# The low part of the second half of an expert's relu values made in two operations, each with a count of its own

## The reference

```python
def _moe2_ref(x, modality_id, w_gate, modality_bias, w1, w2):
    ...
    e_idx = np.argmax(logits, axis=1)
    ...
    for e in range(E):
        mask = e_idx == e
        ...
        h = np.maximum(x[mask] @ w1[e], 0.0)
        out[mask] = gate_w[mask, None] * (h @ w2[e])
```

## Time and profile before

| | |
|---|---|
| median of 3 runs | 618.58 us (618.49 to 619.17) |
| the profiled execution | 619.54 us |
| its span, first to last instruction | 617.7 us |
| mean granted TensorE clock | 0.99 |
| expert stage, 415 to 617.7 us | 202.7 us |
| busy in the whole span | PE 596.2, PEld 498.0, DVE 325.4, ACT 188.1, POOL 125.1 us |
| chain that ended last, by engine | PE 86%, DVE 5%, issue 4%, ACT 2%, DMA 2% |

### The profile page before, as it was taken

How to read it: one execution, slowest core, us unless ns; L and a number is a source line. 1 busy time by engine, 2 the same in 40 slices (tenths; PEclk the granted TensorE clock), 3 DMA queues, 4 the chain that set the end, 5 groups by cost and what they waited for, 6 DMA issues and landing times.

```text
span 617.7 us, 10821 instructions
## 1 busy us (share of the span) xinstructions
PE 596.2 (97%) x3350; PEld 498.0 (81%) x3351; DVE 325.4 (53%) x814; ACT 188.1 (30%) x437; POOL 125.1 (20%) x200
## 2 busy tenths in 40 slices
PE   8999999899999999999999999999999999999996
PEld 4777777788989988899989999877777777777774
DVE  4877787687544464545644577547222228622211
ACT  4988887442010000100000220116222137521121
POOL 5444543996000000000000000010211121211120
PEclk9999999999999999999999999879999999999999
DMA  7865642463010000800010000139311117211110
GB/s 169 182 145 101 145 127 58 133 187 92 1 51 1 1 1 1 314 8 0 0 51 0 0 1 1 51 106 400 125 36 49 34 34 255 72 42 42 34 36 28
DMA packets 76588, 48.09 MB, mean 78 GB/s; under 512 B 54799, under 2 KB 62991, under 8 KB 76560
## 3 DMA queue, kind: packets, MB, share of 16 engines
q1 hardware_dynamic: 72336, 40.03, 22.4%
q0 software_dynamic: 2480, 7.34, 3.6%
q10 hardware_dynamic: 1744, 0.39, 0.3%
HBM read 41.46 MB, written 7.08 MB: 79 GB/s over the span
## 4 chain that ended last, share of the span: by engine, by line
PE 86%; DVE 5%; issue 4%; ACT 2%; DMA 2%; DVEq 1%; SPq 0%; ACTq 0%
PE wide L1160 13%; PE wide L1162 11%; PE wide L1161 11%; PE bank L1160 10%; PE bank L1162 10%; PE bank L1161 10%; PE wide L1148 9%; PE bank L1222 4%; PE wide L1202 3%; PE wide L1327 2%; PE wide L1155 1%; ACT p_sc L501 1%; DMA stage<-in_moe_w 1%; PE bank L1214 1%; DVE h_l L846 1%
## 5 line engine op out<-in xcount | busy, mean ns | idle before, releaser
L843 DVE TENSOR_SCALAR h_act<-bank,alpha_sb 128x384 f32<-128x384 f32 x62 | 38.3, 617 | 109.9 <-PE bank L1162 109.9
L1160 PE MATMUL bank<-x_hl,wts 128*128 (+1 forms) x248 | 85.3, 344 | 0.0
L1162 PE MATMUL bank<-x_hl,wts 128*128 (+1 forms) x248 | 83.5, 337 | 0.0
L1161 PE MATMUL bank<-x_hl,wts 128*128 (+1 forms) x248 | 83.3, 336 | 0.0
L1160 PE MATMUL wide<-wts,h_h 128*128 128x512 f32 x192 | 75.8, 395 | 4.1 <-DVE h_l L846 2.8
L731 POOL DMA_INDIRECT xg<-x_scratch,src_i x16 | 16.7, 1047 | 292.0 <-DVE src_i L1078 256.3
L1162 PE MATMUL wide<-wts,h_l 128*128 128x512 f32 x192 | 75.9, 395 | 0.0
L1161 PE MATMUL wide<-wts,h_h 128*128 128x512 f32 x192 | 75.7, 394 | 0.0
L1160 PE MATMUL wide<-wts,hg_h 128*128 x120 | 51.4, 428 | 5.2 <-DVE hg_l L1114 5.2
L1114 DVE TENSOR_TENSOR hg_l<-wide,hg_h 128x512 fp32r<-128x512 f32 x30 | 20.7, 690 | 64.8 <-ACT hg_h L595 48.9
L1160 PE MATMUL bank<-wts,xg_h 128*128 x120 | 48.7, 406 | 0.5 <-DVE xg_l L1102 0.5
(11 more groups left out here) (203 smaller groups left out, 1021.3 us busy)
## 6 DMA issues: line engine op xcount, KB each, us to landing
stage<-in_moe_w SPq DMA_DIRECT2D x32, 512.0 KB, 6.6
ring<-in_moe_w_in SPq DMA_DIRECT2D x16, 256.0 KB, 2.8
ring<-in_moe_w_out SPq DMA_DIRECT2D x16, 256.0 KB, 2.7
v_raw<-in_v SPq DMA_DIRECT2D x16, 192.0 KB, 2.6
x_scratch<-x2row SPq DMA_DIRECT2D x4, 768.0 KB, 3.5
k_raw<-in_k SPq DMA_DIRECT2D x14, 192.0 KB, 3.0
q_raw<-in_q SPq DMA_DIRECT2D x14, 192.0 KB, 3.3
v_win<-in_v SPq DMA_DIRECT2D x16, 120.0 KB, 2.5
```

The lines of the kernel that those rows point to most:

```text
L843: link(ts(h, acc, 0.0, alpha_sb[:, j:j + 1], ALU.min, ALU.mult))
L1160: pe.matmul(acc, lhs[0], rhs[0], start=start, stop=False)
L1161: pe.matmul(acc, lhs[0], rhs[1], start=False, stop=False)
L1162: return pe.matmul(acc, lhs[1], rhs[0], start=False, stop=stop)
```

## The change

DVE makes the low part of the second half (chunks 4 to 7) in two operations of 256 columns, and each counts `hg_low` up by one; the first half stays one operation with one count. A tile now counts three. PE waits for the first count of the second half before chunks 4 and 5, and for the second before chunks 6 and 7.

```diff
                 def hidden_low(u):
-                    part = lambda x: x[:, 4 * u:4 * u + 4].rearrange("p c t -> p (c t)")
                     dve.wait_ge(hg_high, 2 * t + 1 + u)
-                    tt(part(hg_l), wide[0][:, u * 512:(u + 1) * 512], part(hg_h).bitcast(F32), ALU.subtract
-                       ).then_inc(hg_low, 1)
+                    for c0, c1 in (((4, 6), (6, 8)) if u else ((0, 4),)):
+                        part = lambda x: x[:, c0:c1].rearrange("p c t -> p (c t)")
+                        tt(part(hg_l), wide[0][:, c0 * P:c1 * P], part(hg_h).bitcast(F32), ALU.subtract).then_inc(hg_low, 1)
...
-                pe.wait_ge(hg_low, 2 * t + 1)
+                pe.wait_ge(hg_low, 3 * t + 1)
                 down(range(2))
                 turn_h(t, 1)
                 down(range(2, 4))
-                pe.wait_ge(hg_low, 2 * t + 2)
-                down(range(4, 8))
+                pe.wait_ge(hg_low, 3 * t + 2)
+                down(range(4, 6))
+                pe.wait_ge(hg_low, 3 * t + 3)
+                down(range(6, 8))
```

## The result

| | before | changed |
|---|---|---|
| median | 618.58 us (618.37 to 619.17, 5 runs) | 615.15 us (613.60 to 616.66, 5 runs) |
| ratio | | 0.9931, 95% interval 0.9913 to 0.9948 |
| profiled execution, its span | 619.54, 617.7 us | 616.66, 614.9 us |

The change makes the kernel 3.4 us faster at the medians. Measured again, it gives 614.52 us and a ratio of 0.9924 (0.9910 to 0.9938). The forecast was 613.1 with a range of 611.6 to 616.2: the measured time lies inside it, sign and mechanism hold, and 2 us are missing.

What follows compares the result with a forecast made beforehand. PE, busy for 97% of the span, was taken as the bound, so only its waits could move the time. Gains of 3.82 at chunk 4 and 1.65 at chunk 0 make 5.5: 618.58 - 5.5 = 613.1 us, range 611.6 to 616.2.

Steps and rivals of the forecast that it cites:

- Step 1: PE's wait for chunk 4: the first count comes 0.273 earlier, 14 x 0.273 = 3.8 us gained (0 to 5.4).
- Step 2: Chunks 6 and 7 wait for a count of their own: 0.9 in hand, so no wait, 0 us.
- Step 3, chunk 0: PE's wait for chunk 0: y_copied and hg_low waited for on separate rows, 15 x 0.11 = 1.65 us gained.
- step 4: Tile of 505 to 518 us and the next: VectorE's weight splits carry the time, so the fifteenth 0.273 is lost.
- Rival B: Only the early count helps, nothing is gained at chunk 0: 614.8 us; chance 0.31.
- Step 3, PE's register work: Added register operation L1419 ahead of chunk 6 on PE: taken as 0, at most 15 x 0.11 = 1.7 us lost.
- rival C: PE's queue has no lead; three added instructions cost 0.11 each per tile, 4.95 lost, 619.7 us; chance 0.08.
- The sign that the forecast named: Mean distance of the waits for chunk 4, 13.06, falls by about 0.38 to 12.7.
- Rival D: First count seen only with the pair's end: 0.06 to 0.14 more per tile, 619.5 to 620.8 us; chance 0.03.
- Rival E: PE's loop code no longer at hand at its 14 returns: 15.0 lost, 3.8 gained, 629.8 us; chance 0.03.

Runs made afterwards that it cites:

- e1: The changed kernel, but PE waits for both counts of the second half ahead of chunk 4 and no longer ahead of chunk 6; 618.25 us.
- e3: The kernel before, with PE's wait for y_copied moved ahead of the next tile's transposes; 616.36 us, ratio 0.9955.
- e7: e6 with the wait for y_copied also moved ahead of the next tile's transposes; 610.93 us, ratio 0.9856.
- e2: The kernel before, with one added, always reached wait for hg_low ahead of chunk 6, with a register value of its own; 620.20 us, ratio 1.0016.
- e8: The kernel before, with two added, always reached waits (hg_low and e_low) ahead of chunk 6; 621.56 us.
- e0: The changed kernel run once more, no edit; 614.52 us.
- e9: e7 with the second half made in two operations, the early count on a semaphore of its own, no register instruction added; 609.69 us, ratio 0.9840.
- e6: The kernel before, with the second half's transposes behind chunk 0 instead of behind chunk 1; 612.73 us, ratio 0.9880.
- e5: The changed kernel with its early count on its own semaphore, y_copied waited for early, and operations of 128 and 384 columns; 613.20 us, ratio 0.9902.

## Why the prediction was right, and where its sizes were off

**The mechanism** held in each step that the profile could show. Step 1: the first count comes 0.27 earlier (0.420 for 256 columns where 0.417 was taken from another row of the same form); 15 distances C0 to C4 shrink by 3.99 us together, 0.266 each, against 0.273. The idle at chunk 4 is 0.34 as forecast, and e1 shows that the count alone brings it. The rule of the Trainium skill (VectorE: DVE Perf Modes, "The TRN2 errata") against small operations agrees with the trace as a price: the pair takes 0.76 instead of 0.69, and e1, where PE waits for the whole pair, pays 0.06 per tile for it. It does not decide here, because PE waits for the first part only.

**Step 2**, chunk 6 without a wait, held: no idle of the loads ahead of it.

**Step 3, chunk 0**: 0.11 per tile was taken; the 13 tiles from the second on that don't follow the tile in step 4 give 1.37 us, 0.105 each. e3 shows the cause alone: the place of the wait for `y_copied`. As built this is one instruction less behind the release. Rival B is out for the mechanism, though its 614.8 lies nearer to the medians: the time by itself could not have told it from the forecast.

**Step 3, PE's register work, is the term that was mis-sized.** I put the instruction L1419 at "0, at most 1.7 us lost", because PE issues ahead of itself and the seam's 0.14 looked like the small rest of much hidden work. It costs 0.07 per seam, 0.98 us. The seam's 0.14 was not a rest under a full cover but the sign that the cover had already run out there, since PE has stood still at chunk 4 (e7); e2 and e8 show that what is added then comes through, 0.09 for each instruction. The bound of 0.11 was right in size; to take nothing of it was the error. So rival C was partly true. Of its three instructions only this one counts: L1417 stands where PE waits, and L1413 has taken the place of another instruction and left one less behind the release.

**Step 4**: the gain at chunk 4 of the eighth tile, lost behind DVE's weight splits, is to be seen. H to C0 of the tile after it is 7.79 instead of 7.73, where all the others fell by about 0.1; from the eighth tile's C4 to this C0 it is 10.64 instead of 10.49. The rows that answer to the earlier trace rows:

```profile
515.51 0.76 DVE L1115 TENSOR_TENSOR hg_l<-wide,hg_h 128x256 fp32r<-128x256 f32 x2 [0.18 <-ACT hg_h L601]
516.61 4.63 DVE L964 TENSOR_TENSOR wts<-stage,wts 128x1024 f32 x4 [0.33 <-ACT wts L568]
...
525.90 0.68 DVE L1115 TENSOR_TENSOR hg_l<-wide,hg_h 128x512 fp32r<-128x512 f32 x1
```

The splits still wait 0.33 for ScalarE, so the longer pair does not delay them; DVE's pace from one low part to the other, 516.22 to 526.61 before and 515.51 to 525.90 now, is 10.39 both times.

**The sum**: forecast 5.5, of which 0.11 fall on the first tile's way to C0, outside the table. For the table's stretch that leaves 5.36 of gain; 5.30 were measured (3.99 and 1.31), less 0.98 lost at the seams: 4.32. The sign that the forecast named, the mean distance of the waits for chunk 4, is (605.97 - 427.14) / 14 = 12.77 where it gave 12.7. (Rival D's upper end, 620.8 in the forecast, adds up to 620.7.) Corrected by the seams the forecast would read 614.1, still below both medians, 615.15 and 614.52. For the profiled executions the rest is the time at which the stage is entered: 4.32 less the 1.45 by which the changed kernel reaches the first C0 later gives 2.87, and 619.54 - 616.66 is 2.88; with e0's profile 4.37 and 0.73 sooner give 5.10, and 619.54 - 614.41 is 5.13. For the medians, which have no profiles of their own, this is likely and not shown: the twelve profiles (before, changed, e0 to e9) reach the first C0 between 420.79 and 423.75 us, and nothing ahead of the expert stage was edited in any. Rival E, code that has to be fetched, is out: three packets of instructions move in the stage as before, and no seam of the changed kernel is longer than 0.5.

## What to carry to other kernels

When an engine waits for the end of an operation of which it needs only a part, an earlier count gains just the difference in duration. But look first whether the chain that feeds it can start earlier: here moving the transposes by one chunk gave 7.3 us where the cut gave 4.0. A new semaphore value in a register is not free on an engine whose seam already shows idle time; take values that stand in registers (a second semaphore, if need be). Put a wait that has long been reached ahead of other work, not beside the wait that decides.

## What the runs showed that I had not expected

- Two waits ahead of one register row cost PE about 0.1 us more behind the last release than one wait does (0.34 to 0.37 against 0.23 after DVE's end), although the other semaphore had long been there: as built, the second wait is an instruction of its own. Waiting for it four transposes earlier removes it (e3).
- On PE one register instruction with its wait, behind the last real wait of a tile, lengthens the seam to the next by 0.09 us, two by 0.18 (e2, e8), though six products lie between them and the seam. Where PE has not stood still at chunk 4, the seam has no delay at all (e6, e7, e9).
- A wait that no product and no load visibly waits for can come with 0.12 more at the seam (e5); the reason is only argued.
- The distance from the first chunk 0 to the last chunk 4 repeats within 0.05 us of 182 between two builds, while whole runs of one kernel spread over up to 5 us (the kernel before: 618.61 to 623.56), and between the first profiles of the two kernels the difference arose in the dense layer's first group, from PE's wait for DVE (2.18 us against 1.26) and, behind the longer wait, some 3 us at half the clock. For a change of 1 us the sums over a stage are the better measure.
